# Reordering four partial products of a projection, one VectorE step and three weight splits in a fused attention and two-MLP kernel

## The reference

```python
q_s = softmax(q, axis=-1); k_s = softmax(k, axis=2)        # over features; over tokens
x   = q_s @ (k_s.T @ v)                                    # per head, then joined to 512 columns
h   = gelu_tanh(x @ w_in);  u, v = halves of h             # 512 + 512 columns
v_s = w_sg @ (layernorm(v) * g_ln) + b_sg                  # mixes the 576 tokens
x1  = x + (u * v_s) @ w_out
h2  = relu(x1 @ w_in2); c = 3-tap convolution of h2 over tokens with conv_w
out = (h2 * sigmoid(c)) @ w_out2
```

## Time and profile before

| | |
|---|---|
| time, median of 3 runs | 910.3 us (909.92 to 910.87) |
| time of the profiled execution | 910.3 us |
| its span (first to last instruction) | 908.5 us |
| PE busy | 893.4 us, 98% of the span |
| PEld busy | 831.5 us, 92% |
| DVE busy | 617.7 us, 68% |
| ACT, POOL busy | 398.8 us, 44%; 368.5 us, 41% |
| DMA | 99.59 MB, mean 110 GB/s |

### The profile page before, as it was taken

How to read it: one execution, slowest core, us unless ns; L and a number is a source line. 1 busy time by engine, 2 the same in 40 slices (tenths; PEclk the granted TensorE clock), 3 DMA queues, 4 the chain that set the end, 5 groups by cost and what they waited for, 6 DMA issues and landing times.

```text
span 908.5 us, 15155 instructions
## 1 busy us (share of the span) xinstructions
PE 893.4 (98%) x6132; PEld 831.5 (92%) x6132; DVE 617.7 (68%) x952; ACT 398.8 (44%) x593; POOL 368.5 (41%) x233
## 2 busy tenths in 40 slices
PE   6999999999999999999999999999999999999998
PEld 5799899999999999999999999999999999898986
DVE  7787948678596685875656797767575666757550
ACT  6653554535444445355254354534343343434331
POOL 6673575364572643737132133232232222232220
PEclk9999999999999999999999999999999999999999
DMA  9736673565554645543332202200202020200001
GB/s 299 215 87 232 188 218 116 145 211 177 155 181 135 204 133 154 165 144 83 114 112 75 101 3 86 69 31 12 88 13 87 24 76 24 76 24 24 24 35 47
DMA packets 60037, 99.59 MB, mean 110 GB/s; under 512 B 6720, under 2 KB 25408, under 8 KB 58304
## 3 DMA queue, kind: packets, MB, share of 16 engines
q1 hardware_dynamic: 55360, 89.20, 32.0%
q10 hardware_dynamic: 4608, 9.44, 2.8%
HBM read 78.46 MB, written 19.11 MB: 107 GB/s over the span
## 4 chain that ended last, share of the span: by engine, by line
PE 91%; DVE 3%; POOL 3%; issue 2%; ACT 1%; DMA 0%; POOLq 0%; DVEq 0%; ACTq 0%
PE psum L549 55%; PE psum L541 30%; PE psum L628 2%; PE psum L715 2%; PE psum L665 1%; POOL plain_arena L1839 1%; POOL plain_arena L1821 1%; PE psum L587 1%; POOL plain_arena L1882 0%; DVE split_arena L1571 0%; DMA plain_arena<-in_kT 0%; DVE split_arena L1563 0%; DVE plain_arena L1322 0%; DVE plain_arena L1470 0%; DVE plain_arena L1371 0%
## 5 line engine op out<-in xcount | busy, mean ns | idle before, releaser
L549 PE MATMUL psum<-split_arena 128*128 128x288 f32 x4032 | 555.9, 296 | 1.2 <-DVE split_arena L1456 0.5
L549 PEld LDWEIGHTS psum<-split_arena 128*128 128x128 f32 x4032 | 545.2, 189 | 8.0 <-issue 1.6
L541 PE MATMUL psum<-split_arena 128*128 128x512 f32 x1248 | 294.3, 390 | 0.2 <-DVE split_arena L1456 0.2
L541 PEld LDWEIGHTS psum<-split_arena 128*128 128x128 f32 x1248 | 230.6, 188 | 46.7 <-DVE split_arena L1456 0.6
L1961 POOL TENSOR_TENSOR plain_arena<-plain_arena 128x576 f32<-128x576 f32 x64 | 107.7, 1683 | 279.2 <-ACT plain_arena L1081 279.2
L1592 DVE SCALAR_TENSOR_TENSOR plain_arena<-plain_arena 128x576 f32<-128x576 f32 x64 | 96.2, 1503 | 2.3
L1587 DVE TENSOR_SCALAR plain_arena<-plain_arena 128x576 f32<-128x576 f32 x64 | 36.0, 563 | 86.7 <-ACT plain_arena L1075 86.7
L1075 ACT ACTIVATE plain_arena<-psum 128x576 f32<-128x576 f32 x64 | 41.7, 651 | 106.6 <-PE psum L549 68.9
L1871 POOL TENSOR_TENSOR plain_arena<-plain_arena 128x2 f32<-128x2 f32 (+1 forms) x24 | 20.4, 852 | 126.6 <-DVE plain_arena L1487 126.6
L1882 POOL TENSOR_TENSOR plain_arena<-plain_arena 128x576 f32<-128x576 f32 x32 | 48.9, 1529 | 52.2 <-DVE plain_arena L1526 52.2
L1081 ACT ACTIVATE plain_arena<-plain_arena 128x576 f32<-128x576 f32 x64 | 43.7, 683 | 42.6 <-DVE split_arena L1765 39.5
(11 more groups left out here) (107 smaller groups left out, 780.9 us busy)
## 6 DMA issues: line engine op xcount, KB each, us to landing
x_dram<-plain_arena ACTq DMA_DIRECT2D x32, 288.0 KB, 2.1
plain_arena<-x_dram SPq DMA_DIRECT2D x8, 1152.0 KB, 6.2
out_rows<-plain_arena SPq DMA_DIRECT2D x36, 256.0 KB, 2.0
plain_arena<-in_kT SPq DMA_DIRECT2D x7, 1152.0 KB, 5.2
plain_arena<-in_k SPq DMA_DIRECT2D x7, 1024.0 KB, 7.0
plain_arena<-in_v SPq DMA_DIRECT2D x28, 256.0 KB, 4.2
plain_arena<-in_q_heads SPq DMA_DIRECT2D x6, 1152.0 KB, 8.2
split_arena<-q_max_dram SPq DMA_DIRECT2D x12, 576.0 KB, 6.4
```

Of the source, the lines that this page charges most:

```text
L541: mm = e.matmul(out, stat[s], mov[m], start=first and n == 0, stop=last and n == 2, skip_group_check=True)
L549: mm = e.matmul(out[:, h, 0:NH], stat[s], mov[m][:, h * NH:(h + 1) * NH], start=first and n == 0, stop=last and n == 2, skip_group_check=True)
```

## The change

It has five edits. (1) TensorE, every body: the first two contraction blocks of output blocks 0 and 1, then block 2 of 0 and 1, then blocks 0 to 2 of output block 2, then the last contraction block of all three; before, each step went over all three output blocks. (2) VectorE, bodies 1 to 6: `lo_q_rows(a, 1)` stands in front of `lo_g(m, 2)` instead of behind it. (3) SyncE: the wait for the x1 stores in front of the load of W2 piece 0 is gone. (4) SyncE, ScalarE, VectorE, body 7: `hi_w2(0)` and `hi_w2(1)` stand in front of `hi_x(7, 2)`, `hi_w2(2)` follows behind it instead of behind the last `gelu_u`, and `lo_w2(2)` stands with `lo_w2(0)` and `lo_w2(1)` in front of the LayerNorm's `moments` instead of behind its `normalise`. (5) SyncE: `move_tail(7)` stands in front of piece 6 instead of piece 5.

```diff
--- before.py
+++ after.py
@@ -506,12 +506,10 @@
 
 
             e.wait_ge(q_lo, q_lows(B))
-            for x in x1_out:
-                e.wait_ge(x, 32 * (B - 2) + 16)
             for n, (src, hi, lo) in enumerate(W2):
                 if n == 3:
                     load_x2(0)
-                if n == 5:
+                if n == 6:
                     move_tail(B - 1)
                 if n >= 3:
                     e.wait_ge(w2_lo, n - 2)
@@ -823,9 +821,12 @@
                         kv_piece(a, 2)
                         kv_piece(a, 3)
 
-                for fs in ([0, 1], [2], [3]):
-                    for d in range(DT - 1):
+                for fs in ([0, 1], [2]):
+                    for d in range(2):
                         o_part(m, d, fs)
+                o_part(m, 2, [0, 1, 2])
+                for d in range(DT - 1):
+                    o_part(m, d, [FT - 1])
                 if a is not None:
                     x_piece(a, 0)
                 else:
@@ -1142,11 +1143,13 @@
                     if a is not None:
                         hi_q(a, j)
 
+                if a is None:
+                    hi_w2(0)
+                    hi_w2(1)
                 if not start:
                     hi_x(m, DT - 2)
                 if a is None:
-                    hi_w2(0)
-                    hi_w2(1)
+                    hi_w2(2)
                 if late:
                     exp_q(a, 0)
                     exp_k(a, 0)
@@ -1182,7 +1185,6 @@
                         hi_vn(m, 2)
                 if a is None:
                     e.wait_ge(u_done, B * FT)
-                    hi_w2(2)
                     hi_w2(3)
                     hi_w2(4)
                 if start:
@@ -1659,7 +1661,7 @@
                     max_k(n, 0)
                     max_k(n, 1)
                 elif a is None:
-                    for w in range(2):
+                    for w in range(3):
                         lo_w2(w)
                 if start:
                     moments(m, 1)
@@ -1701,7 +1703,6 @@
                     tile(4)
                 else:
                     if a is None:
-                        lo_w2(2)
                         lo_w2(3)
                     affine(m, 0)
                     lo_g(m, 0)
@@ -1714,9 +1715,10 @@
                     if a is not None:
                         lo_kv(a)
                     affine(m, 3)
+                    if a is not None:
+                        lo_q_rows(a, 1)
                     lo_g(m, 2)
                     if a is not None:
-                        lo_q_rows(a, 1)
                         lo_q_rows(a, 2)
                     else:
                         lo_w2(W2_LATE)
```

## The result

The changed kernel takes 915.91 us (median of 6 runs, 915.07 to 918.02) against 910.41 us before (6 runs, 909.11 to 911.50): a ratio of 1.0063, 95% interval 1.005 to 1.0078. The direction was forecast, the size was not: +3.1 us and 911.2 to 915.2 us were predicted. The profiled execution took 916.24 us.

The account below looks back on a forecast made before the run. TensorE was taken as the bound, busy 98% of the span and all of each loop period. The terms -0.69 + 6 × 0.57 + 0.4 = +3.1 us on 910.3 us gave 913.4 us, range 911.2 to 915.2.

Parts of the forecast that it names:

- Edit 1 in body 0: Body 0, output block 2: TensorE's wait on `lo_kv` goes and no new one comes; gain 0.69 us.
- Edits 1 and 2 in bodies 1 to 6: `lo_g(m, 2)`, slowed beside `gate(3)`, comes 0.40 us late; with restart 0.57 us per body, 3.4 us in six.
- the due time: Projection of bodies 1 to 6: `lo_g(m, 2)` is first used behind 24 matmuls, 3.20 us after the start.
- Edit 3: Body 6 into 7: early weight loads gain nothing but delay the stores; TensorE waits 0 to 0.7 us, 0.4 taken.
- the second rival: End of body 6: stores land after 6.3 us, wait 2.3 us instead of 0.4, total 915.3 us; chance 8%.
- the landing of the store: Body 6's first store beside the early loads: taken to land after 4.0 to 4.7 us.
- the prediction's own chain: Late store delays `add_x(6, 2)`, then `add_x(6, 3)`'s half steps, then TensorE in body 7; wait 0 to 0.7 us.
- The prediction's estimate of about 3 us to landing: Body 6's store, given half the bandwidth by alternating queues, lands after about 3 us at no cost; not relied on.
- Edit 4: Body 7: earlier splits on ScalarE and a third `lo_w2` on VectorE fit into idle time; cost nothing.
- the cover: Body 7, ScalarE: the moved splits' data has been there for 2 us and more, so they cost nothing.
- Edit 5: SyncE, body 7: piece 5 loads 18 us earlier, the tail copy behind it waits for GpSimd anyway; cost nothing.

Follow-up runs that it names:

- e11: The kernel before with the new matmul order in body 0 alone; 910.08 us, ratio 0.9997.
- e1: The changed kernel with `lo_g(m, 2)` back in front of `lo_q_rows(a, 1)` on VectorE; 915.30 us, ratio 1.0047.
- e4: The kernel before with only `lo_q_rows(a, 1)` moved in front of `lo_g(m, 2)`, old matmul order kept; 910.75 us, ratio 1.0002.
- e8: The e7 kernel with GpSimd's `gate(3)` of bodies 1 to 6 also waiting for `lo_g(2)`; 911.98 us, ratio 1.0019.
- e2: The changed kernel with SyncE's wait for the x1 stores back in front of the weight loads; 915.88 us, ratio 1.0063.
- e7: The kernel before with the swapped VectorE subtractions and the new matmul order in bodies 1 to 7 only; 913.88 us, ratio 1.0040.
- e5: The kernel before with only SyncE's wait for the x1 stores removed; 915.97 us, ratio 1.0061.
- e6: The changed kernel with `lo_g` first again and the x1-store wait put between the weight loads and the 1152 KB load; 910.58 us, ratio 1.0001.
- e9: The kernel before with only the first weight pieces' splits moved in front of `hi_x(7, 2)` on ScalarE; 912.07 us, ratio 1.0023.
- e10: The kernel before with only the new matmul order, in all bodies; 909.95 us, ratio 0.9995.
- e3: The changed kernel with `lo_g` first again and the x1-store wait back in front of the weight loads; 911.67 us, ratio 1.0014.

## Why the prediction was wrong in size

**Edit 1 in body 0: right.** Forecast -0.69, measured -0.61 in the changed kernel and -0.65 in e11, and in e11 no new wait in its place. In the changed kernel's trace a wait of 0.4 us on `lo_x` stands behind it, at the start of body 1.

**Edits 1 and 2 in bodies 1 to 6: right in cause, place and, for five bodies, size.** The second place beside `gate(3)` costs 1.99 us (forecast 2.00), the due time was 24 matmuls behind the start, the wait adds 0.54 us per body (forecast 0.57). e1, e4 and e8 show the parts: undo the order of the subtractions, keep the old due time, or keep GpSimd away, and the waits are gone. Body 1 was given 0.57 and shows 1.02 in the profiled execution, because its `gate(2)` started later: GpSimd first stood 2.17 us for a DMA, against 1.01 before.

```profile
129.49 2.81 POOL L1834 TENSOR_TENSOR plain_arena<-plain_arena,split_arena 128x576 f32<-128x576 f32 x2 [2.17 <-DMA split_arena<-q_rec_dram]
```

In e2 and e7 the six waits sum to 3.1 us, none above 0.5, so this is one execution's DMA and not the change. e7 as a whole, +3.4 us by its medians, is the forecast of this step. The Trainium skill, page "SBUF — State Buffer", section "Who interferes with whom", says that a VectorE instruction with two SBUF inputs contends with a GpSimd instruction that reads SBUF, and that the order of issue decides which of them stands. The traces agree: the second to issue took 1.99 us, and in e8, apart in time, 0.75. The subtraction that stood ended 0.6 us behind GpSimd's end, though, and not the full 0.75.

**Edit 3: the step that failed.** The mechanism was named (stores behind the early loads), its price was set at 0.4 us, with 2.3 as the worst (the second rival, given 8%); it was 2.0 us in the changed kernel and 5.5 us in e5. The term that was mis-sized is the landing of the store, put at 4.0 to 4.7 us. I took it from a store issued together with the same loads (4.7 us) and argued that loads older than the store would be mostly through. The three weight pieces were (the last landed 1.4 us after the store's issue), the 1152 KB load wasn't: it ended 5.4 us after the store's issue, and the store landed just behind it, after 5.8 us here and 7.0 in e1 and e5. With 5.8 us in place of 4.7 the prediction's own chain gives a wait of 1.8 us, near the 1.98 measured. e6 shows that it is this load.

The store isn't always behind that load: in the trace before, the fourth store of batch 6 was issued 0.04 us after it, took 6.3 us, and landed 2.7 us ahead of its end.

```profile
449.33 0.48 SPq L505 DMA_DIRECT2D plain_arena<-x_dram  x1
449.37 0.37 ACTq L1016 DMA_DIRECT2D x_dram<-plain_arena  x1
```

The losses of e5 (+5.5) and e7 (+3.4) don't add, they make +5.5 and not 8.9. In the changed kernel the wait in body 6, just ahead of it, put the store 3.4 us behind the large load instead of 2.8, and the large load took 8.8 us instead of 9.7 or 9.8 (why isn't shown), so TensorE stood for less. It also lost nothing to the clock: where it stood for 3.3 us or more (e1, e5) the granted clock fell to 0.50 and the slow matmuls added 1.7 and 2.9 us to the loss, which the prediction hadn't counted; in the changed kernel's profiled execution it stood for 1.8 us and the clock stayed at 1.00.

The Trainium skill, page "DMA: Bandwidth & Descriptors", section "Queues, rings and completion order", says that a DMA engine goes round between the queues for which it has work. The trace agrees from 452.1 us on, where packets of both queues moved in the same stretch. The prediction's estimate of about 3 us to landing, worked out from that rule, misses the 4.0 us before the store's first packet (4.2 us in e1, 4.4 in e5). Why the first packet came so late, no run here settles.

**Edit 4: costed at nothing, right only beside edit 3.** In the changed kernel nobody waits for it. By itself it costs 1.7 us (e9), which I hadn't priced: the cover was the early load, and the prediction should have said so.

**Edit 5:** TensorE waits for it in no run that has it; no run tests it alone.

**What the sum leaves.** -0.61 + 0.34 + 1.02 + 2.70 + 1.98 - 0.49 = +4.94 us between the first projection and the end, and +1.01 before it. The latter is not the change: the code up to there is the same in all 14 traces, and the projection of body 0 starts anywhere between 75.4 and 77.0 us in them (75.89 before, 76.92 after). Open are the 0.34 us at the start of body 1, which some executions have and others haven't (e10 and e11), and the pace of part of body 7, where some executions get up to 0.6 us ahead of the others without a wait less. Open too is a part of the median: with body 1 at 0.54 us, as in e2 and e7, the parts that the runs show come to -0.61 + 6 × 0.54 + 1.98 = 4.6 us, and the medians differ by 5.5.

## What to carry to other kernels

When TensorE is the bound and never waits, price an edit by due times: date each waited-for value against the matmul that uses it, and give each place in a queue the duration that this place has, not the one that the operation has elsewhere. Two edits that are free alone can cost together, and a wait that looks idle may keep a large load away from a small store that someone needs: before removing it, list what will be in flight and, as a bound, let the store land behind all of it. Keep the wait, or put it in front of the large transfer alone.

## What the runs showed of the hardware

A 288 KB store from ScalarE's queue, issued 2.8 to 3.4 us after a 1152 KB load from SyncE's, moved its first packet 4.0 to 4.4 us after its issue and landed within 0.4 us of that load's end, 5.8 to 7.0 us after its issue (changed kernel, e1, e5). Undisturbed the two times are 0.8 and 2.1 us. Issued together with that load, in the trace before, a store took 6.3 us but landed 2.7 us ahead of it.

A VectorE subtraction with both inputs in SBUF took 1.99 us instead of 0.75 when it started 0.5 us behind GpSimd's `gate`; `gate` took 1.88 us instead of 1.43 when a VectorE subtraction had started first.

Around the end of a TensorE wait of 3.3 to 3.5 us (e1, e5) the granted clock fell to 0.50, the level of 1.2 GHz, for 3.4 and 6.8 us, and six matmuls of 288 columns took 1.64 us instead of 0.95. Behind waits of 1.5 to 2.4 us (changed kernel, e2, e3, e9) it stayed at 1.00.
